# Moving loads, first splits and two weight halves around the phase changes of a two-layer FFN kernel, and making its last step by output halves

## The reference, cut to what matters

```python
# q, k, v: (4, 8, 576, 64); keys and values averaged over groups of 8
x = attention(q, mean8(k), mean8(v))      # (2304, 512) tokens x model
h = x @ w1_in                             # (2304, 2048)
g = where(h >= 1, h, where(h <= -1, 0, (h + 1) ** 2 / 4))
x = g @ w1_out                            # (2304, 512)
h = x @ w2_in
g = maximum(h, 0) + log1p(exp(-abs(h)))   # softplus
out = g @ w2_out                          # (2304, 512)
```

## Time and profile before

| | |
|---|---|
| median of 3 executions | 898.89 us (897.16 to 899.85) |
| the profiled execution, its own time | 899.97 us |
| its span in the trace | 898.2 us |
| TensorE busy | 850.6 us, 95% |
| VectorE busy | 633.7 us, 71% |
| ScalarE busy | 455.8 us, 51% |
| GpSimd busy | 413.0 us, 46% |
| mean granted TensorE clock | 0.974 of full speed |
| DMA over the span | 187 GB/s |

### The profile page before, as it was taken

The page is one execution under the profiler, slowest core; times in us unless marked ns, Lnnn a source line. Parts: engine busy times, 40 slices in busy tenths (PEclk is TensorE's granted clock), DMA queues, the critical chain, the costliest instruction groups (busy, mean ns, idle before and its releaser), DMA issues.

```text
span 898.2 us, 12875 instructions
## 1 busy us (share of the span) xinstructions
PE 850.6 (95%) x4986; PEld 831.4 (93%) x4986; DVE 633.7 (71%) x670; ACT 455.8 (51%) x667; POOL 413.0 (46%) x297
## 2 busy tenths in 40 slices
PE   7876899999999998999999998999999699999997
PEld 6664699999999998999999998999999699999997
DVE  4999656544444678768766689788788988669642
ACT  3786543222213334433444785887777544444542
POOL 7998227556544542124000389698657542221000
PEclk8998799999999999999999999999999799999999
DMA  8974127567465697454552254566554787555532
GB/s 195 201 183 121 29 85 223 191 219 234 161 215 200 204 323 281 178 211 146 206 188 82 81 181 141 202 205 203 202 193 168 248 314 272 193 211 199 193 118 71
DMA packets 106137, 167.79 MB, mean 187 GB/s; under 512 B 21856, under 2 KB 94048, under 8 KB 101472
## 3 DMA queue, kind: packets, MB, share of 16 engines
q1 hardware_dynamic: 101280, 162.28, 54.8%
q10 hardware_dynamic: 4800, 4.72, 1.6%
HBM read 96.21 MB, written 70.78 MB: 186 GB/s over the span
## 4 chain that ended last, share of the span: by engine, by line
PE 76%; DVE 8%; ACT 5%; POOL 4%; DMA 4%; issue 2%; SPq 1%; DVEq 0%; ACTq 0%
PE ps L1046 38%; PE ps L1064 33%; DMA ops<-gops 3%; DVE xs L847 2%; PE ps L990 1%; DVE v_sum L769 1%; PE ps L1017 1%; POOL ops L508 1%; POOL ops L503 1%; POOL ops L511 1%; ACT qT L569 1%; PE ps L1077 1%; DVE ops L903 1%; DMA q_raw<-in_q_dram 1%; POOL ops L505 1%
## 5 line engine op out<-in xcount | busy, mean ns | idle before, releaser
L1046 PEld LDWEIGHTS ps<-xs,W 128*128 128x128 f32 x2304 | 401.9, 189 | 5.5 <-POOL W L496 3.8
L1046 PE MATMUL ps<-xs,W 128*128 128x384 f32 x2304 | 403.6, 336 | 3.1 <-POOL W L496 3.1
L1064 PE MATMUL ps<-xs,Tm 128*128 128x384 f32 x2016 | 358.8, 338 | 13.7 <-DVE xs L847 13.7
L1064 PEld LDWEIGHTS ps<-xs,Tm 128*128 128x128 f32 x2016 | 354.2, 190 | 15.3 <-DVE xs L847 8.7
L627 ACT ACTIVATE xs<-ops 128x768 fp32r<-128x768 f32 (+1 forms) x148 | 111.7, 826 | 175.5 <-PE ps L1064 155.0
L503 POOL TENSOR_TENSOR ops<-ops 128x384 f32<-128x384 f32 x48 | 65.3, 1360 | 244.3 <-DVE ops L903 138.1
L847 DVE TENSOR_TENSOR xs<-ops,xs 128x768 fp32r<-128x768 f32 (+1 forms) x148 | 160.0, 1141 | 9.4 <-ACT xs L627 9.4
L646 ACT ACTIVATE t_a<-t_a 128x768 f32<-128x768 f32 x48 | 40.8, 850 | 138.6 <-DVE t_a L872 138.6
L872 DVE TENSOR_SCALAR t_a<-ps 128x768 f32<-128x768 f32 x48 | 45.9, 956 | 86.8 <-PE ps L1046 86.5
L916 DVE TENSOR_TENSOR X<-ps,X 128x768 f32<-128x768 f32 x42 | 39.6, 955 | 88.2 <-PE ps L1064 88.2
L903 DVE TENSOR_TENSOR ops<-t_a,t_b 128x768 f32<-128x768 f32 x48 | 62.4, 1300 | 32.3 <-ACT t_b L666 32.0
(11 more groups left out here) (57 smaller groups left out, 690.8 us busy)
## 6 DMA issues: line engine op xcount, KB each, us to landing
gops<-ops SPq DMA_DIRECT2D x48, 1344.0 KB, 5.8
ops<-gops SPq DMA_DIRECT2D x36, 1536.0 KB, 7.2
X<-gops SPq DMA_DIRECT2D x22, 384.0 KB, 6.3
w_raw<-in_moe_w_in_dram SPq DMA_DIRECT2D x32, 256.0 KB, 4.0
t_raw<-in_moe_w_out_dram SPq DMA_DIRECT2D x6, 1024.0 KB, 9.3
k_raw<-in_k_dram SPq DMA_DIRECT2D x16, 288.0 KB
q_raw<-in_q_dram SPq DMA_DIRECT2D x32, 144.0 KB, 5.8
v_raw<-in_v_dram SPq DMA_DIRECT2D x16, 288.0 KB
```

The source lines that it names most:

```text
L1046: last = mm(banks[:, tb, :], W[:, slot, f, part, c * P:(c + 1) * P], x[:, x_part, at:at + TB], start=c == 0 and s == 0, stop=c == KC - 1 a ...
L1064: last = mm(banks[:, d, :], Tm[:, t, part, j, d * P:(d + 1) * P], g[:, g_part, at * TB:(at + 1) * TB], start=at == 0 and s == 0, stop=at = ...
```

## The change

Five edits. The operations are the same, except that the last step's add, copy, transpose and store are made in two halves.

- **First splits.** The four pieces of the first fill of the product phase are made at quads 17 to 20 (`FIRST_AT = QUADS - JJ + 1 = 17`), one each, on ScalarE and VectorE, in both layers.
- **First load.** `load_ops(layer, NT)` stands before the store of quad 23.
- **Third raw block.** `load_raw(layer, 2)` stands after the third `load_ops`.
- **Last weight halves.** In layer 1, `hi_w` of the last two slots is made at quads 0 and 1 (it was at 2 and 3), `lo_w` on GpSimd at quads 1 and 2, ahead of the sums (it was after the sums of quads 3 and 4).
- **Last step.** It is made by output halves, with the transposes of step 19 between them.

```diff
@@ sync @@
+                    if k == QUADS - 1:
+                        load_ops(layer, NT)
                     store_ops(layer, k)
...
-                    if k >= QUADS - 3:
+                    if QUADS - 3 <= k < QUADS - 1:
                         load_raw(layer, k - QUADS + 3)
-                for m in range(NT, STEPS):
+                for m in range(NT + 1, STEPS):
                     load_ops(layer, m)
+                    if m == NT + SLOTS - 1:
+                        load_raw(layer, 2)
@@ gpsimd @@
+                    if layer == 1 and 1 <= k < 3:
+                        lo_w(1, W_LATE + k - 1)
                     s_sums(layer, k)
-                    if layer == 1 and W_LATE <= k + 3 < JJ:
-                        lo_w(1, k + 3)
@@ scalar @@
-                    if layer == 1 and W_LATE <= k + 4 < JJ:
-                        hi_w(1, k + 4)
-                    if k >= QUADS - 2:
-                        for piece in range(2 * (k - QUADS + 2), 2 * (k - QUADS + 2) + 2):
-                            fill_hi_piece(fill_of(layer, NT), piece)
+                    if layer == 1 and k < 2:
+                        hi_w(1, W_LATE + k)
+                    if 0 <= k - FIRST_AT < PIECES:
+                        fill_hi_piece(fill_of(layer, NT), k - FIRST_AT)
...
-                if layer == 1:
-                    copy_y(STEPS - 1)
-                    store_out(STEPS - 1)
+            for d in range(2):
+                last_half(d)
@@ vector @@
-                    if k >= QUADS - 2:
-                        for piece in range(2 * (k - QUADS + 2), 2 * (k - QUADS + 2) + 2):
-                            fill_lo_piece(fill_of(layer, NT), piece)
+                    if 0 <= k - FIRST_AT < PIECES:
+                        fill_lo_piece(fill_of(layer, NT), k - FIRST_AT)
...
+                    if layer == 1 and m == STEPS + 1:
+                        for d in range(2):
+                            add_half(d)
@@ tensor @@
+            def last_product(d):
...
+                for at, j in enumerate(W_ORDER[1]):
...
+                    for s, (part, g_part) in enumerate(((0, 0), (1, 0), (0, 1))):
+                        last = mm(banks[:, d, :], Tm[:, t, part, j, d * P:(d + 1) * P],
...
+                last.then_inc(half_done, 1)
...
-            turn_y(STEPS - 1)
+            last_product(0)
+            turn_y(STEPS - 2)
+            last_product(1)
+            for d in range(2):
+                turn_half(d)
```

More of the change, by code:

```diff
@@ L68 @@
 W_LATE = JJ - 2
+FIRST_AT = QUADS - JJ + 1
 W_TURNS = ((), (0, 1), (2, 3, 4), (5,))
@@ L445, in _ @@
             for o in range(OUT_BUFS):
-                sp.wait_ge(out_stored[o], 16 * (len(turn_number) // OUT_BUFS))
+                sp.wait_ge(out_stored[o], 16 * sum(1 for t in range(len(turn_number) - 1) if t % OUT_BUFS == o))
+            for d in range(2):
+                sp.wait_ge(out_half[d], 16)
         @block.gpsimd
@@ L917, in add_y, with add_half @@
                                                 ).then_inc(y_added, 1)
+            def add_half(d):
+                p, i = divmod(STEPS - 1, NT)
+                (tb, n, other), = Y_OPS[p]
+                dve.wait_ge(half_done, d + 1)
+                dve.wait_ge(y_added, y_count(1, STEPS - 1) - 1)
+                nc.vector.tensor_tensor(x_block(i, tb, n)[:, d, :], bank_pair(v_of_step[2 * STEPS - 1])[:, d, :],
+                                        x_block(i, *other)[:, d, :], ALU.add).then_inc(half_added, 1)
             dve.wait_ge(kT_zero, 1)
@@ L1067, in product, with turn_half @@
                 last.then_inc(step_done, 1)
+            def last_product(d):
+                p, i = divmod(STEPS - 1, NT)
+                fill, n = fill_of(1, NT + STEPS - 1), 2 * STEPS - 1
+                banks, g, t = bank_pair(v_of_step[n]), xs[fill % 2], t_buf(1, p)
+                pe.wait_ge(*banks_free(v_of_step[n]))
+                for at, j in enumerate(W_ORDER[1]):
+                    if at % 2 == 0:
+                        pe.wait_ge(*fill_done(fill, at // 2))
+                    for s, (part, g_part) in enumerate(((0, 0), (1, 0), (0, 1))):
+                        last = mm(banks[:, d, :], Tm[:, t, part, j, d * P:(d + 1) * P],
+                                  g[:, g_part, at * TB:(at + 1) * TB],
+                                  start=at == 0 and s == 0, stop=at == JJ - 1 and s == 2)
+                last.then_inc(half_done, 1)
+            def turn_half(d):
+                m = STEPS - 1
+                (tb, n), i = FINAL_OF[m // NT], m % NT
+                banks = bank_pair(v_of_turn[m])
+                pe.wait_ge(*banks_free(v_of_turn[m]))
+                pe.wait_ge(half_added, d + 1)
+                for s in range(TB // P):
+                    last = nc.tensor.transpose(banks[:, d, s * P:(s + 1) * P],
+                                               x_block(i, tb, n)[:, d, s * P:(s + 1) * P], ident[:, :])
+                last.then_inc(half_turned, 1)
             def turn_y(m):
@@ L1108, in _ @@
                     make_h(layer, a)
-                for m in range(STEPS):
+                for m in range(STEPS if layer == 0 else STEPS - 1):
                     product(layer, m)
```

19 lines of the change are left out of this document (18 added, 1 removed).

## The result

| | before | after |
|---|---|---|
| median, 4 runs each on one chip | 898.02 us (895.52 to 899.85) | 887.31 us (885.78 to 889.24) |
| the profiled execution, its own time | 899.97 us | 888.39 us |
| its span | 898.2 us | 885.9 us |

The ratio is 0.9884, with a 95% interval from 0.9849 to 0.9918. The change is faster, beyond its interval: by 10.7 us where 20.2 were forecast. The median is 1.3 us above the upper end of the forecast range.

A forecast was written before the change was run, and what follows sets the result against it. TensorE was taken to bound the kernel, losing time to waits and clock falls. Gains 7.18 + 4.85 + 7.31 + 0.8 = 20.1 us from 899.97 leave 879.8; with the median 1.08 lower, 878.7 us, range 873.5 to 886.

The forecast's parts named there:

- Layer 0's change: Start of layer 0's products: earlier activation load removes both step 3 waits and the clock fall behind them, gaining 7.18 us.
- Five microseconds to spare: cost nil: Late third raw block: product 2's splits done at 355, step 6 due at 360.3, so no cost in either layer.
- The weight halves: Layer 1's first token block: earlier splits of the last two weight slots remove two GpSimd waits and a clock fall, 4.85 us.
- Layer 1's change: From layer 1's h phase to its products: 12.36 us lost, 5.05 left (wait before step 1, clock fall), gain 7.31 us.
- There VectorE is idle 1.34 us a quad before a total and a piece takes 0.95 to 1.77: Layer 1, quads 17 to 20: early first-fill pieces fit, so step 0 starts with the h phase's end, at 697.8.
- VectorE does not get through in time: Rival, layer 1's change: early pieces leave VectorE behind; last total no earlier gives 881.4, all four pieces late 885.8; chance 0.25.
- The exclusive lock: Shared GpSimd/VectorE port, layer 1's change: pieces every 2.6 us, gain about 2.7 smaller; judged contradicted by pieces of 1.42 us.
- The end: Last step in halves: store issued 0.4 us sooner and landing in 2.9 us, together 0.8 us, bounds -0.4 and 1.7.
- The slower rival: Third raw block so late that step 6 waits in both layers, 26 us from issue to landing; 902 or more, chance 0.03.
- the load was not held: Rival, both changes: full DMA engines land the earlier load no sooner, 7.18 + 1.2 stay lost, 887.1; chance 0.05.

The follow-up runs named there:

- run 7: Changed kernel with both load moves undone (first activation load behind the last store, third raw block at its old place): 890.64 us, ratio 0.9913.
- run 1: Changed kernel with the third raw block loaded at its old place, the early activation load kept: 881.23 us, ratio 0.9847.
- run 2: Changed kernel, but GpSimd's sum for product 3 waits until VectorE has split step 6's fill; raw block stays late: 880.03 us, ratio 0.9817.
- Run 10: Changed kernel with layer 1's last two weight slots split at their old place on ScalarE and GpSimd: 891.98 us, ratio 0.9944.
- run 12: Changed kernel with layer 1's four early low pieces two columns wide, the rest of step 0's low half left out: 884.87 us (2 runs), ratio 0.9878.
- run 8: Changed kernel with product 0's Tm two quads earlier, layer 1's early low pieces on GpSimd, GpSimd's product 3 sum behind step 6's fill: 880.22 us, ratio 0.9783.
- run 9: As run 8, plus layer 1's step 1 fill between pairs 45 and 46 and step 0's copies behind step 2's fill: 879.8 us, ratio 0.9802.
- run 4: Changed kernel with layer 1's step 1 fill made between the third-last and second-last total, ScalarE's half likewise a pair later: 886.82 us, ratio 0.9889.
- run 3: Changed kernel with layer 1's four early low pieces made by GpSimd instead of VectorE: 882.39 us, ratio 0.9862.

## Where the prediction was right and where it failed

- **Layer 0's change: right but for step 6.** The load issued at 315.35, and step 3 without its waits and its clock fall, are as forecast, and run 7 confirms it. The step that failed is "Five microseconds to spare: cost nil". 3.8 us were there for `Tm` (ready at 357.5, due at 361.26). What I did not follow is who else is touched by the late sums: two of them moved onto step 5's fill and made step 6's start late, and the third then held its first piece for 4.70 us. Price 1.92 us here and 2.37 in layer 1; runs 1 and 2 show the cause.
- **The weight halves: right.** 5.07 against 4.85. Run 10 shows that 3.11 of it are waits; the clock behind them may or may not fall, so that the close agreement is in part luck.
- **Layer 1's change: the large miss, 1.54 against 7.31.** The step that failed is "There VectorE is idle 1.34 us a quad before a total and a piece takes 0.95 to 1.77": from this I let three of the four pieces cost nothing. They do fit by their own time, but the operations behind them then ran beside GpSimd's sums and took 1.77 and 1.64 in place of 0.95 and 1.30. The last total came 13.0 us after h, not 10.3 (run 12: 9.9 without the pieces). That makes step 1's wait 4.92 and not 3.35, plus 0.45 for a bank at step 0; it is the rival "VectorE does not get through in time", at its first stage (it said a wait of 5.2 us, and 881.4). Its clock fall was 2.8 us against 1.70 taken from a shorter wait, and the 2.37 of step 6 come on top. Forecast left 5.05, measured 10.55. The median lies beyond this rival's worst case too, because no rival held the waits at step 6, 4.29 us in both layers, with weights that come in time.
- **The exclusive lock.** GpSimd's sums held VectorE's two-input pieces: 9.73 us for four pieces beside two sums, 7.31 beside one, 3.55 alone. I had let the 1.42 us a piece of the earlier trace rows speak against a lock "in full". That was a wrong reading of a mean: one by one, these six pieces took 0.95, 1.76, 1.75, 1.75, 1.76 and 0.94 us, the four slow ones beside sums, and the sums took 1.61 to 1.72 where the same sums take 1.01 alone. It looks as if each waited for the other in turn. Beside a sum of 4.6 us the first piece waits it out. The Trainium skill (SBUF — State Buffer, "Who interferes with whom") gives the shared port as an exclusive lock; the traces agree (4.70 us for one piece), and its warning was to be applied wherever a long GpSimd operation moves, not only where I looked.
- **The end: right in kind.** 0.3 us sooner by path, where 0.4 was forecast; that the stage gave 1.12 for 0.8 is luck, since the landing varies by more than the gain. The bounds of this term, -0.4 and 1.7, do not follow from its own sizes, which give -0.7 and 1.4. In this trace the eleven stores of 384 KB of line 707 landed in 3.2 us (median; the shortest 2.6) and the two of 192 KB in 2.1. The Trainium skill (DMA: Bandwidth & Descriptors, "Anatomy of one DMA") gives, as an estimate from its figures, 0.45 us for this halving. Its figures are fitted to DMAs that GpSimd issues, and these stores are issued by ScalarE; the rows give 0.5 against the shortest and 1.1 against the median.
- **The slower rival** did not come near: its raw block landed in time, and the load was not held.

The runs also point to a better version. Run 2, one wait of GpSimd on top of the change, has a median of 880.03 us, run 8 has 880.22 and run 9 879.80; the intervals of runs 8 and 9 lie wholly below that of the change, run 2's overlaps it in part. What stays open is step 1's wait, 3.6 to 5 us in every complete kernel with an early first fill and step 1's fill behind the last total (2.59 in run 12). In no order that I tried did the wait go: runs 4 and 9 only handed it on. So it seems to take less VectorE work around the change; no complete kernel here tried that.

## What to carry to other kernels

Idle time of an engine that shares a port with another is not free time: look at what the operations behind the inserted one will then run beside, and count their lengthening too. When a transfer is put later, follow what it releases to its end, including the long operations of other engines that then fall on somebody's critical work; a wait that keeps a long GpSimd operation off a critical VectorE one can be worth more than the move itself. And when the first consumer of a saturated engine is served, expect the wait at the next one.

## What I had not expected of the hardware

- **The clock after a short wait is not settled by the wait's length.** It held after 1.92, 2.26, 2.37, 2.59, 2.68 (at least for the 12 matmuls up to the next wait) and even 3.22 us (run 4: the 48 matmuls behind it took 8.58), and fell after 2.00, 2.28, 2.38, 2.40 and 2.63. Such a fall costs 1.6 to 1.7 us. A term for it is a chance, not a sum.
- **Behind a long wait the price differs too**: after 4.92 and 4.95 us the mean clock of the next 6.1 us was 0.54 and 0.64, after 4.32 (run 3) 0.53 and after 4.07 0.72. That is 2.8, 2.2, 2.9 and 1.7 us lost, for the same matmuls.
- **The part of the program that no kernel here changes spread most**: attention ended so variously that the first product matmul began at 302.96 to 311.60 us, always 195.63 us after the same h phase matmul, so a difference of whole spans below some 8 us says little by itself.
